# First piece of a fused convolution and feed-forward kernel: sums by TensorE, an on-chip identity, and other owners for the early preparation

## The reference

```python
# x: (4, 4096, 192), weight_gen: (4, 4096, 8, 7)
w = exp(weight_gen - max(weight_gen, axis=-1)); w = w / (sum(w, axis=-1) + 1e-9)
x_pad = concatenate([zeros((B, 6, 192)), x], axis=1)
y[b, s, h, g] = sum over k of w[b, s, h, k] * x_pad[b, s + k, h, g]     # 8 heads of 24 columns
h = y.reshape(16384, 192) @ w_in         # w_in: (192, 2048)
g = h * (1 / (1 + exp(-1.702 * h)))
out = g @ w_out                          # w_out: (2048, 192)
```

## Time and profile before

| | us |
|---|---|
| median of 3 runs | 1127.0 (1126.95 to 1127.77) |
| the profiled execution | 1126.67 |
| its span | 1124.9 |
| TensorE matmul busy | 1111.5 (99%) |
| VectorE busy | 802.1 (71%) |
| ScalarE busy | 622.0 (55%) |
| GpSimd busy | 12.8 (1%) |

### The profile page before, as it was taken

One profiled execution on the slowest core, in us unless ns is written; L12 is line 12 of the kernel. 1 busy time (PEld: TensorE's weight loads), 2 busy tenths in 40 slices (PEclk: granted clock), 3 DMA queues, 4 the chain that ended last, 5 costly groups with the idle time before them and its releaser, 6 DMA issues.

```text
span 1124.9 us, 21696 instructions
## 1 busy us (share of the span) xinstructions
PE 1111.5 (99%) x9748; PEld 915.3 (81%) x9748; DVE 802.1 (71%) x710; ACT 622.0 (55%) x661; POOL 12.8 (1%) x13
## 2 busy tenths in 40 slices
PE   6999999999999999999999999999999999999998
PEld 4888888888888888888888888888888888888886
DVE  7999988687685966859668496785858768587322
ACT  7767655464645555455464554645555555454543
POOL 2100000000000000000000000000000000000000
PEclk9999999999999999999999999999999999999999
DMA  8801010101001010010100101010010100100000
GB/s 274 238 15 54 15 54 1 39 29 40 29 2 39 29 40 29 1 57 12 40 29 18 51 1 40 29 40 29 1 40 29 40 29 1 40 29 1 29 1 29
DMA packets 9980, 43.46 MB, mean 39 GB/s; under 512 B 1120, under 2 KB 2400, under 8 KB 7584
## 3 DMA queue, kind: packets, MB, share of 16 engines
q1 hardware_dynamic: 8400, 40.51, 10.9%
q0 software_dynamic: 1488, 1.57, 0.9%
HBM read 24.77 MB, written 12.58 MB: 33 GB/s over the span
## 4 chain that ended last, share of the span: by engine, by line
PE 98%; DVE 1%; DMA 0%; issue 0%; ACTq 0%; DVEq 0%; SPq 0%; ACT 0%
PE hid L655 47%; PE acc_main L671 31%; PE acc_rest L671 21%; DMA gate<-in_x_first 0%; DVE hid L489 0%; DVE prod L483 0%; PE acc_main L622 0%; DVE hid L483 0%; DVE outs_main L511 0%; ACTq L73 0%; DVE outs_rest L552 0%; DVEq L73 0%; PE acc_rest L622 0%; SPq L199 0%; ACT outs_main L304 0%
## 5 line engine op out<-in xcount | busy, mean ns | idle before, releaser
L317 ACT ACTIVATE gate<-hid 128x1024 f32<-128x1024 f32 x256 | 263.1, 1028 | 480.0 <-PE hid L655 479.4
L568 DVE TENSOR_TENSOR gate_lo<-gate,gate_hi 128x1024 fp32r<-128x1024 f32 x256 | 312.9, 1222 | 260.6 <-ACT gate_hi L320 260.5
L655 PE MATMUL hid<-xt,w_hi 64*128 64x512 f32 x3072 | 431.5, 386 | 0.0
L655 PEld LDWEIGHTS hid<-xt,w_hi 64*128 64x128 f32 x3072 | 287.7, 184 | 61.6 <-ACT gate_hi L320 0.8
L671 PE MATMUL acc_main<-gate_hi,w 64*128 64x512 f32 x2048 | 315.8, 386 | 0.0
L320 ACT ACTIVATE gate_hi<-hid 128x1024 fp32r<-128x1024 f32 x256 | 260.7, 1018 | 0.0
L671 PEld LDWEIGHTS acc_main<-gate_hi,w 64*128 64x128 f32 x2048 | 191.9, 184 | 40.3
L655 PE MATMUL hid<-xt,w_lo 64*128 64x512 f32 x1536 | 215.8, 386 | 0.0
L671 PE MATMUL acc_rest<-gate_hi,w 64*128 64x512 f32 x1024 | 199.6, 386 | 0.0
L671 PE MATMUL acc_rest<-gate_lo,w 64*128 64x512 f32 x1024 | 199.6, 386 | 0.0
L671 PE MATMUL acc_main<-gate_lo,w 64*128 64x512 f32 x1024 | 199.6, 386 | 0.0
(11 more groups left out here) (57 smaller groups left out, 229.7 us busy)
## 6 DMA issues: line engine op xcount, KB each, us to landing
xwin<-in_x_runs SPq DMA_DIRECT2D x15, 1056.0 KB, 4.9
out<-outs_main SPq DMA_DIRECT2D x13, 512.0 KB, 2.6
out<-outs_rest SPq DMA_DIRECT2D x13, 256.0 KB, 2.9
taps<-in_tap_runs SPq DMA_DIRECT2D x1, 3136.0 KB, 10.4
taps<-in_w_rows SPq DMA_DIRECT2D x2, 1536.0 KB, 9.6
w_hi<-w_hi SPq DMA_DIRECT2D x2, 768.0 KB, 10.4
w_lo<-w_lo SPq DMA_DIRECT2D x2, 768.0 KB, 8.7
out<-outs_main SPq DMA_DIRECT2D x6, 256.0 KB, 2.0
```

The source lines that it names most:

```text
L317: nc.scalar.activation(gate[:, v % 2, :, :], hid[:, v % 2, :, :], ACT.Gelu_apprx_sigmoid).then_inc(gate_ready, 1)
L568: nc.vector.tensor_tensor(gate_lo[:, v % SLOTS, :, :], gate[:, v % 2, :, :], gate_hi[:, v % SLOTS, :, :], ALU.subtract).then_inc(gate_lo_r ...
L655: last = nc.tensor.matmul(hid[:, v % 2, h, :], w[rows, k if j else slice_of(h, k), q, f], xt[rows, j % 2, part, k, :], start=(i == 0), sto ...
```

## The change

Eight edits, all but one in what happens before the first eight units are through.

- **Identity.** No longer an input. GpSimd writes ones and masks them (`affine_select`); it also writes zeros into a part of `gate_lo`. The warm-up is 16 matmuls of 128x128 zeros that wait for these only.
- **Sums.** TensorE adds VectorE's first product (columns 0 to 511) and all of GpSimd's three products in PSUM, by matmuls with the identity (`pile`, into `head_pile`). GpSimd's sum is dropped and its third product cut into two halves. VectorE sums its other products, the last 256 columns of the first among them, into `head_sum`, and then adds `head_pile` and `head_sum` by slice, four times, the repeated slice 0 among them.
- **Turned slices.** ScalarE copies all three; VectorE only subtracts.
- **Unit 0** takes w1_hi and w1_lo for slice 0, then for slice 1, then for slice 2, and the remainders last.
- **Gate copied.** For units 0 and 8, `gate_hi` is a rounded copy of `gate` rather than a second gate on `hid`, and first product n + 2 waits for `gate` only.
- **w1 remainders.** `LATE` shrinks from 512 to 256 of 1024 columns: VectorE makes the other 256 after unit 1, together with w2 chunks 2 and 3 (before after unit 2).
- **w2.** ScalarE rounds chunks 0 and 1 before the units, 2 and 3 after unit 0, 4 and 5 after unit 2 and 6 and 7 after unit 3, each of the last two followed by its negation; GpSimd's DMAs for the second pair wait for the second.
- **Pieces 1 and 2** have their maxima, shifts and exponentials in one instruction each, and the 20 steps of piece 0's units are spread as 0, 5, 3, 2, 2, 2, 4, 2 in place of 0, 6, 2, 4, 2, 2, 2, 2.

```diff
-NEG_AT, ADDED_AT = 2, (5, 6)
+NEG_AT, ADDED_AT = (2, 3), (5, 6)
+W1_ADDED_AT = 4
-STEPS_AT = ((0, 6, 2, 4, 2, 2, 2, 2),
+STEPS_AT = ((0, 5, 3, 2, 2, 2, 4, 2),
-WARM_UP = 4
+WARM_UP = 16
...
-        LATE = slice(FH // 2, FH)
+        LATE = slice(FH * 3 // 4, FH)
+        GATE_COPIED = (0, UNIT0[1])
...
-            sp.dma_start(ident[:], identity).then_inc(ident_loaded, 16)
...
-            act.wait_ge(head_summed, 1)
-            nc.scalar.activation(head_conv[:, :, SLICES, :], head_conv[:, :, 0, :], ACT.Copy).then_inc(head_again, 1)
-            for k in (0, 2):
+            for k in range(SLICES):
                 act.wait_ge(head_turned_ready, k + 1)
-                nc.scalar.activation(xt[:, 0, 0, k, :], head_turned[k], ACT.Copy).then_inc(head_hi_act, 1)
+                nc.scalar.activation(xt[:, 0, 0, k, :], head_turned[k], ACT.Copy).then_inc(head_hi, 1)
             act.wait_ge(w2_loaded, 16)
-            for at in (0, 2):
-                round_w2(at, at + 2)
+            round_w2(0, 2)
...
+                    if n in GATE_COPIED:
+                        act.wait_ge(gate_ready, n + 1)
+                        nc.scalar.activation(gate_hi[:, v % SLOTS, :, :], gate[:, v % 2, :, :], ACT.Copy
+                                             ).then_inc(gate_hi_ready, 1)
...
-                        round_w2(4, CH // 2)
+                        round_w2(2, SOON)
...
-                    if n in (2, 4):
-                        at = slice((n + 2) * P, (n + 4) * P)
+                    if n == W1_ADDED_AT:
                         act.wait_ge(w1_added, 16)
-                        nc.scalar.activation(w1_lo[:, :, 0, at], w1_raw[:, :, at], ACT.Copy).then_inc(w1_late_ready, 1)
+                        nc.scalar.activation(w1_lo[:, :, 0, LATE], w1_raw[:, :, LATE], ACT.Copy).then_inc(w1_late_ready, 1)
...
+                    if n in NEG_AT:
+                        at, to = LATE_CHUNKS[NEG_AT.index(n)]
+                        round_w2(at, to)
+                        act.wait_ge(w2_hi_ready, to // 2)
+                        nc.scalar.activation(w2_of(at, to, slice(D, 2 * D)), w2_of(at, to, slice(0, D)).bitcast(F32),
+                                             ACT.Copy, scale=-1.0).then_inc(w2_negated, 1)
...
-                mul(0, head_acc)
-                mul(1, head_prod[0])
+                mul(0, head_prod[0])
+                mul(1, head_acc)
                 mul(2, head_prod[1])
+                mul(3, head_prod[2])
+                dve.wait_ge(head_op, 7)
+                add(head_acc, head_acc, head_prod[1])
+                dve.wait_ge(head_op, 9)
+                add(head_acc[:, N:N_FIRST], head_acc[:, N:N_FIRST], head_prod[0][:, N:N_FIRST])
+                dve.wait_ge(head_op, 10)
+                add(head_sum, head_acc, head_prod[2])
                 dve.wait_ge(head_op, 11)
+                dve.wait_ge(head_piled, 1)
+                for k in range(SLICES + 1):
+                    a, b = (z.rearrange("p (u a k c) -> p u a k c", a=2, k=SLICES, c=32)[:, :, :, k % SLICES, :]
+                            for z in (head_pile, head_sum))
...
-            dve.wait_ge(head_turned_ready, 2)
-            nc.vector.tensor_copy(xt[:, 0, 0, 1, :], head_turned[1]).then_inc(head_hi_dve, 1)
...
-                        maxima_and_shift(1)
-                        maxima_and_shift(2)
-                    if n == 2:
+                        maxima_and_shift(1, 2)
+                    if n == 1:
+                        w1_remainder(slice(4 * P, 6 * P))
                         w2_remainder(2, SOON)
...
+            nc.gpsimd.memset(zeros, 0.0).then_inc(zeros_ready, 1)
+            nc.gpsimd.memset(ident[:], 1.0).then_inc(ident_ones, 1)
+            pool.wait_ge(ident_ones, 1)
+            nc.gpsimd.affine_select(ident[:], ident[:], pattern=[[-1, P]], compare_op=ALU.is_equal, fill=0.0, base=0,
+                                    channel_multiplier=1).then_inc(ident_ready, 1)
...
+                pe.wait_ge(zeros_ready, 1)
+                for _ in range(WARM_UP):
+                    nc.tensor.matmul(head_turned[0][:, 0:P], zeros, zeros, start=True, stop=True)
+                FORE, AFT, WAY = slice(0, N), slice(N, N_FIRST), N_FIRST // 2
...
+                pe.wait_ge(ident_ready, 1)
+                pe.wait_ge(head_op, 5)
+                pile(head_prod[0], FORE, start=True)
+                pe.wait_ge(shared_op, 1)
+                pile(shared_prod[0], FORE)
+                pile(shared_prod[0], AFT, start=True)
+                pe.wait_ge(shared_op, 2)
+                pile(shared_prod[1], FORE)
+                pile(shared_prod[1], AFT)
+                pe.wait_ge(shared_op, 3)
+                pile(shared_prod[2], slice(0, WAY))
+                pe.wait_ge(shared_op, 4)
+                pile(shared_prod[2], slice(WAY, N), stop=True)
+                pile(shared_prod[2], AFT, stop=True).then_inc(head_piled, 1)
...
-                wait(pe, gate_hi_ready, n - 1)
+                if n - 2 in GATE_COPIED:
+                    pe.wait_ge(gate_ready, n - 1)
+                else:
+                    wait(pe, gate_hi_ready, n - 1)
...
+                if n == 0:
+                    terms = [(w, 0, k) for k in range(SLICES) for w in (w1_hi, w1_lo)] + terms[2 * SLICES:]
```

More of the change, by code:

```diff
@@ L33 @@
 CROSS_HI_AT, CROSS_LO_AT = (7, 7, 5), (7, 7, 5)
-WARM_UP = 4
+WARM_UP = 16
 SHARED = 3
 def ffn_of_dynamic_conv(nc: bass.Bass, x_runs: bass.AP, tap_runs: bass.AP, x_first: bass.AP, tap_first: bass.AP,
-                        identity: bass.AP, w1_rows: bass.AP, w2_rows: bass.AP, out: bass.AP):
+                        w1_rows: bass.AP, w2_rows: bass.AP, out: bass.AP):
     CB = x_runs.shape[2]
@@ L108, in ffn_of_dynamic_conv @@
         x_head = gate[:].rearrange("p b h n -> p (b h n)")[:, 0:FIRST_WIN * D].rearrange("p (t d) -> p t d", d=D)
-        head_prod = [prod[:, k, 0:N_FIRST] for k in range(2)]
-        shared_prod = [prod[:, 0, N_FIRST:N_CONV], prod[:, 1, N_FIRST:N_CONV], conv[:, 0:N_FIRST]]
+        head_prod = [prod[:, 0, 0:N_FIRST], prod[:, 0, N_FIRST:N_CONV], prod[:, 1, 0:N_FIRST]]
+        head_sum = prod[:, 1, N_FIRST:N_CONV]
+        shared_prod = [conv[:, 0:N_FIRST], conv[:, N_FIRST:N_CONV], head_more[:]]
+        zeros = gate_lo[:, 0, 0, 0:P].bitcast(F32)
         head_flat = outs_main[:].rearrange("p h n -> p (h n)")
@@ L259, in _, with exponentials @@
         def _(act):
-            def exponentials(j):
-                act.wait_ge(taps_shifted, j + 1)
-                nc.scalar.activation(taps[:, tap_span(j, j)], taps[:, tap_span(j, j)], ACT.Exp).then_inc(taps_exped, 1)
+            def exponentials(j, last=None):
+                last = j if last is None else last
+                act.wait_ge(taps_shifted, last + 1)
+                nc.scalar.activation(taps[:, tap_span(j, last)], taps[:, tap_span(j, last)], ACT.Exp
+                                     ).then_inc(taps_exped, last + 1 - j)
             def round_piece(j):
@@ L606, in turn_head, with pile @@
             def turn_head():
-                flat = x_head.rearrange("p t d -> p (t d)")
-                pe.wait_ge(x_loaded, 16)
-                pe.wait_ge(head_op, 5)
-                for i in range(WARM_UP):
-                    nc.tensor.matmul(hid[:, 0, 0, :], flat[:, i * P:(i + 1) * P], flat[:, N:2 * N], start=True, stop=True)
-                pe.wait_ge(ident_loaded, 16)
+                pe.wait_ge(zeros_ready, 1)
+                for _ in range(WARM_UP):
+                    nc.tensor.matmul(head_turned[0][:, 0:P], zeros, zeros, start=True, stop=True)
+                FORE, AFT, WAY = slice(0, N), slice(N, N_FIRST), N_FIRST // 2
+                def pile(part, cols, start=False, stop=False):
+                    return nc.tensor.matmul(head_pile[:, cols], ident[:], part[:, cols], start=start, stop=stop)
+                pe.wait_ge(ident_ready, 1)
+                pe.wait_ge(head_op, 5)
+                pile(head_prod[0], FORE, start=True)
[10 more added lines that the diff above has]
+                pile(shared_prod[2], AFT, stop=True).then_inc(head_piled, 1)
                 for k in range(SLICES):
-                    if k < SLICES - 1:
-                        pe.wait_ge(head_summed, k + 2)
-                    else:
-                        pe.wait_ge(head_again, 1)
+                    pe.wait_ge(head_summed, k + 2)
                     for u in range(FIRST):
@@ L740 @@
         "tap_first": wg.reshape(runs, run, h * k)[:, 0:NARROW].reshape(P, head * h * k),
-        "identity": _np.eye(P, dtype=x.dtype),
         "w1_rows": w_in.reshape(2, SLICES, 32, 2, f // 2).transpose(3, 0, 2, 1, 4).reshape(P, SLICES, f // 2),
```

97 lines of the change are left out of this document (39 added, 58 removed).

## The result

The changed kernel takes **1124.80 us** (median of 22 runs, 1124.53 to 1125.52) against 1126.87 (22 runs, 1126.68 to 1127.77): a ratio of 0.9982, interval 0.9976 to 0.9988. By that bound the two kernels count as the same. Its profiled execution took 1124.66 us with a span of 1122.9; before it was 1126.67 with 1124.9.

A forecast was written before the change was run, and what follows sets the result against it. TensorE was taken as the bound, busy 1111.5 of 1124.9 us. Gains of 1.48 + 0.43 + 0.28 + 0.28 - 0.07 = 2.4 gave span 1122.5, profiled 1124.3, median 1124.6 us; 8-in-10 range 1123.7 to 1126.4.

The forecast's parts named there:

- A: Whole kernel: the forecast outcome, 1124.1 to 1125.0 us, chance 0.58, of which 0.4 below 1124.75.
- the border: Whole kernel: 1124.75 us, 0.2% (2.25 us) below 1127.0; only a time below it counts as faster.
- B: Whole kernel: gain partly given back by late clock rise, accumulating DMAs or remainder 14; 1125.0 to 1125.7 us, chance 0.27.
- its own signs: Head, units 1, 2 and 10: matmuls near 14.3 and 16.4, no second-gate waits; wrong if piles end after 12.3.
- First product: Head: sums by slice from 12.0, transposes 12.88, first copy 13.54, first matmul 14.31, 1.48 us earlier.
- Unit 1: Start of unit 1: slice copies and unit 0's new order bring it to 16.43 from 18.34, another 0.43 us gained.
- The holes: Units 2 and 10: copied gates remove waits for ScalarE's second gate, 0.28 us gained at each.
- Preparation: First eight units: gate 2's second until 26.5, piece 1 transposed by 44.8, 1.75 earlier; accumulating DMA landing at 42.0.
- Rival B's second cause: First eight units: accumulating DMAs land no earlier, and the stream loses 0.9 us.
- The leak: Remainder 14 and piece 2's x window: slack used up, 0.07 us taken off, at most 0.5.
- B's first cause: Head: the clock rises only as the warm-up ends (7.8), so piles end 0.85 us later.
- D's point of decision: Head: a clock rise after about 10.9 us makes the kernel slower; low through the piles, 1130 to 1131, chance 0.05.

The follow-up runs named there:

- gates_twice: Changed kernel with the second gate taken from PSUM for units 0 and 8 as for all others, no gate copied: 1124.87 us.
- window_first: Changed kernel with the x window of piece 2 issued ahead of the taps of the wide pieces in SyncE's queue: 1124.46 us.
- window_first_steps: Changed kernel with the x window of piece 2 issued before the wide pieces' taps, and one VectorE step moved behind remainder 14: 1124.51 us.
- vector_sums: Changed kernel without piles: VectorE and GpSimd make the head's sums as before, warm-up again four matmuls on x: 1126.45 us.
- warm_24: Changed kernel with 24 warm-up matmuls on zeros in place of 16: 1126.33 us.
- no_warm_up: Changed kernel without its 16 warm-up matmuls on zeros: 1126.64 us.
- ident_loaded: Changed kernel with the identity loaded by DMA behind w1 and w2 instead of made by GpSimd; zeros and warm-up stay: 1133.16 us.
- before_window_first: Kernel before the change, with only the x window of piece 2 issued ahead of the wide pieces' taps: 1126.86 us.
- best: Changed kernel, x window issued first, head x in two DMAs, VectorE adding GpSimd's second product's last 256 columns, w1's negated copy later: 1124.26 us.

## Why the prediction was right

The time was 0.2 us from the forecast, inside A's own range, and each step can be set beside its row. Two things have to be said first. Part of the closeness is luck: the gain forecast was 2.4 us and the medians have 2.07, but the kernel before came out at 1126.87 where the forecast had started from 1127.0, which hides 0.13 of the difference. And of the three outcomes it had given "faster" the most, 0.52, and "same" came, with 0.42; with a forecast 0.15 us from the border that was little more than a coin. (Its 0.52 also counts "a little of B", though all of B, from 1125.0 up, lies above the border.)

By its own signs it was not clean either. The first matmul came at 14.77 and not near 14.3, unit 1 at 16.96 and not near 16.4. The last pile stands in the timeline until 12.39 (10.93 + 1.46), past the 12.3 that it had named as wrong; by the 4.73 us of the sum the piles end at 12.20. And a wait of 0.2 between 20 and 85 us is new, the one for remainder 14. What follows says what each of them cost.

**First product.** Forecast at 14.31, found at 14.77 (the timeline: `PE L677 MATMUL` for the x slices at 14.77), 0.46 late. Two things make it up. x landed 0.32 later in this profile (6.32 against 6.00); over all profiles with the old order of loads it runs from 6.00 to 6.70, and 0.07 of it is systematic: SyncE's first issue is at 0.80 or 0.81 in every kernel in which GpSimd makes the mask, 0.74 in all others. And the piles took 5.24 from the end of VectorE's first product (7.27) to the sums by slice (12.51), where the sum had 5.04 (6.96 to 12.0). The 4.73 for 2816 columns fits between; mis-sized was the joint ahead of them, 0.20 from the product to the first matmul (7.47), which the sum had put at nothing. Behind them 0.31 passed, as much as the sum had left in all. It is no accident of one run: gates_twice and window_first show the same 6.19 from VectorE's first product to the sums. From the sums on, the working holds within 0.08: transposes 0.80 behind them (forecast 0.88), first copy 1.50 (1.54), first matmul 2.26 (2.31).

**Unit 1.** Forecast 0.43 of further gain: unit 1 comes 2.19 after the first matmul, where 2.12 was forecast and 2.55 stood before. Together 16.96 against 18.34: 1.38 us in place of 1.91, or 1.70 with x's landing taken out.

**The holes.** Unit 2 follows unit 1 after 2.04, so its 0.28 came in full; units 8 to 10 give 0.31 where 0.28 was forecast. 1.38 + 0.28 + 0.31 = 1.97, the 2.0 of the two spans. gates_twice says that not all of the two holes reaches the median.

**Preparation.** Gate 2's second ended at 27.01 (forecast 26.5, the head being 0.5 later) and no weight load waited for it. Piece 1 was transposed at 44.45 in place of 45.59, 1.14 earlier and not the 1.75 forecast. ScalarE no longer waited for the accumulating DMA at all: its copy ran at 40.31, where the sum had it not before 42. Rival B's second cause was therefore no danger, and the term was too careful.

**The leak.** Forecast 0.07, at most 0.5. In the profile it is as small as that:

```profile
57.20 0.96 DVE L414 TENSOR_TENSOR conv<-xwin,tap_norm 128x768 f32<-128x768 f32 x1
79.57 0.74 PE acc_main L693 x6
```

The window, issued at 44.44 and 12.7 on its way, was there at 57.1, and VectorE took it at 57.20 without a wait: no slack was left. Remainder 14 shows a wait of 0.2, which costs the chain 0.06 (six such matmuls take 0.68 elsewhere). The medians say more. window_first lies 0.30 to 0.34 below the changed kernel, and the same swap does nothing to the kernel before. window_first_steps, with the swap too, has the same median as window_first within 0.05. So **the window seems to take some 0.3 us** of the gain in the median. How, is argued and not seen: in the profiles of vector_sums and warm_24 the window landed 13.9 and 14.3 after its issue and cost VectorE 1.19 and 1.56, and some executions of the changed kernel may be of that kind, but its one profile isn't. The forecast had the place and the bounds right and a value near the low end, because it priced the landing by one row of before, 12.4.

**Clock.** The rise came at about 6.8 to 6.9 (the loads of the warm-up are 0.21 apart and 0.33 long up to the one at 6.56; the one at 6.91 takes 0.19), where 5.4 was supposed: 5.8 us after the first matmul and not 4.4. The loads of the warm-up then ended at 7.44 and not at 6.7, just behind VectorE's first product (7.27). It cost nothing yet: window_first, where TensorE stood for 1.11 us between warm-up and piles, has the same 6.19 to the sums. B's first cause was near, all the same. D's point of decision, 10.9, was far. no_warm_up shows its mechanism and its price, warm_24 that more zeros are no cure.

**The sum.** With x's landing out, the span gained 2.32 where 2.40 was forecast. The medians have 2.07; the 0.07 of the later issue and the window can fill the difference, which I can't divide further. Against its own before the kernel keeps 0.22 without the piles, 0.03 without the warm-up and 1.06 with the old preparation. These losses add up to more than the gain, so no edit has a price by itself.

**Open.** No run took away unit 0's new order or ScalarE's three slice copies: that they gave unit 1's 0.36 rests on the rows of one profile. Why the window, issued 1.15 earlier than before, lands no sooner after its issue than 12.7, and in two kernels 14, isn't settled: the load of the taps ahead of it now starts while the copies of w1 between halves, issued at 34.7 and 8.0 us long, are still running, but no run took that overlap away. Nor do I know why a mask instruction on GpSimd moves the first issue of SyncE by 0.07.

## What to carry to other kernels

Where one engine is full from some point on, price a change by when that point begins and by the holes behind it; and take the landing of the first input out of each span before comparing two profiles, for it alone moved them by up to 0.7 us. When the front comes forward by two microseconds, go through every transfer that is issued at a fixed distance ahead of its use: here the small window behind a large load was left without slack, and swapping the two issues, worthless before, gave 0.3 us in the medians. A matmul with an identity adds in PSUM while VectorE multiplies, but at the low level of the clock it costs twice as much (0.86 in place of 0.43 for a pass of 512 columns), and that is where TensorE was after standing for 2.73 us. So the warm-up has to reach nearly up to the data, and no further: 24 matmuls in place of 16 held up the piles.

## What the runs showed of the hardware

- **The rise of TensorE's clock**, by the length of its weight loads, came about 3 us after its first matmul (ident_loaded and warm_24: 0.33 long still at 3.51 and 3.79, 0.19 at 3.90 and 4.14), 3.5 (no_warm_up), up to 4.4 (before), 5.8 (after), and in two profiles with the warm-up of before not within 5.3 us (before_window_first, vector_sums). The loads of the same 32 passes of zeros took 4.99 us in ident_loaded and 6.44 in best.
- **After standing idle** for 2.73 us and 7.86 us it began at the low level again; in window_first, after 1.11, it did not. The granted clock read 1.00 through all of it: in these stretches only the length of a load (0.34 or 0.19) and its spacing tell.
- **A small transfer beside a large one** in another queue landed 5.3 us after its issue; ahead of it in the same queue, 2.0. Here the order within one queue kept the small one short.
- **GpSimd** filled 128x128 fp32 in 0.20 and masked it in 0.29 us, and a 128x768 product took 1.50; that the products started 0.03 ahead of VectorE's shows that neither the mask nor the fills held them up.
